# A convolution feeding two gated layers: the first two tiles convolved in PSUM with paired tails, and weight blocks split where they are first needed

## What is computed

```python
x_pad = np.concatenate([np.zeros((B, pad, D)), x], axis=1)
out = np.einsum('hk,bskhg->bshg', softmax(weight), x_unf)   # 7 taps
h = x @ w_in;  g = h * np.cos(h);                          x = g @ w_out   # layer 1
h = x @ w_in2; g = h * np.clip(h + 3.0, 0.0, 6.0) / 6.0;   out = g @ w_out2 # layer 2
```

## Time and profile before

| | us |
|---|---|
| median of 3 runs (2280.49 to 2280.93) | 2280.5 |
| the profiled execution | 2280.99 |
| its span, first to last instruction | 2279.3 |
| TensorE busy | 2245.0 (98%) |
| VectorE busy | 1811.7 (79%) |
| ScalarE busy | 1722.4 (76%) |
| GpSimd busy | 1509.4 (66%) |

### The profile page before, as it was taken

One profiled execution on the slowest core, in us unless ns is written; L12 is line 12 of the kernel. 1 busy time (PEld: TensorE's weight loads), 2 busy tenths in 40 slices (PEclk: granted clock), 3 DMA queues, 4 the chain that ended last, 5 costly groups with the idle time before them and its releaser, 6 DMA issues.

```text
span 2279.3 us, 56966 instructions
## 1 busy us (share of the span) xinstructions
PE 2245.0 (98%) x19560; PEld 1842.9 (81%) x19560; DVE 1811.7 (79%) x2509; ACT 1722.4 (76%) x2836; POOL 1509.4 (66%) x1059
## 2 busy tenths in 40 slices
PE   7899999999999999999999999999999999999998
PEld 5688888888888888888888888888888888888886
DVE  8778877888877887878888778888778878788753
ACT  5867777777777777777777777777777777777774
POOL 6766666667666667666666666676666676666664
PEclk9999999999999999999999999999999999999999
...
DMA packets 208245, 33.04 MB, mean 14 GB/s; under 512 B 203088, under 2 KB 207184, under 8 KB 208208
## 3 DMA queue, kind: packets, MB, share of 16 engines
...
## 4 chain that ended last, share of the span: by engine, by line
PE 94%; DVE 3%; ACT 2%; issue 0%; SPq 0%; DMA 0%; DVEq 0%; ACTq 0%
PE h_ps L390 45%; PE acc L397 30%; PE acc_tail L404 20%; ACT pre L562 1%; DVE gate L669 1%; DVE pre L658 1%; ACT g_hi L569 1%; DVE in_ftail L717 1%; DVE in_f L717 1%; ACT pre L552 0%; DVE in_tail L730 0%; DMA blk_tail<-in_x 0%; SPq L333 0%; ACT wout L598 0%; ACT in_hi L581 0%
## 5 line engine op out<-in xcount | busy, mean ns | idle before, releaser
L824 POOL TENSOR_TENSOR g_lo<-gate,g_hi 128x512 fp32r<-128x512 f32 x1024 | 1469.0, 1456 | 722.2 <-ACT g_hi L569 721.8
L397 PE MATMUL acc<-g_hi,wout 64*128 64x512 f32 x4096 | 1421.9, 387 | 1.7 <-POOL g_lo L824 1.7
L397 PEld LDWEIGHTS acc<-g_hi,wout 64*128 64x128 f32 x4096 | 755.0, 184 | 84.8 <-issue 3.4
L390 PE MATMUL h_ps<-in_hi,win_hi 64*128 64x512 f32 x2048 | 798.7, 391 | 11.8 <-DVE in_tail L730 10.7
L404 PE MATMUL acc_tail<-g_lo,wout 64*128 64x512 f32 x2048 | 797.6, 389 | 0.0
L390 PE MATMUL h_ps<-in_lo,win_hi 64*128 64x512 f32 x2048 | 792.9, 387 | 0.0
L390 PE MATMUL h_ps<-in_hi,win_lo 64*128 64x512 f32 x2048 | 792.9, 387 | 0.0
L390 PE MATMUL h_ps<-in_tail,wtail_hi 64*128 64x512 f32 x2048 | 792.7, 387 | 0.0
L404 PE MATMUL acc_tail<-g_hi,wout 64*128 64x512 f32 x2048 | 792.4, 387 | 0.0
L397 PE MATMUL acc<-g_lo,wout 64*128 64x512 f32 x2048 | 791.7, 387 | 0.0
L569 ACT ACTIVATE g_hi<-gate 128x512 fp32r<-128x512 f32 x1024 | 616.7, 631 | 116.0 <-DVE gate L672 56.8
...
## 6 DMA issues: line engine op xcount, KB each, us to landing
x_in<-in_x SPq DMA_DIRECT2D x128, 64.0 KB, 2.2
out_dram<-o_blk SPq DMA_DIRECT2D x128, 64.0 KB, 1.8
...
```

The costliest lines, as they stand in the source:

```text
L390: return pe.matmul(chunk_of(h_ps, q, half), w, x, start=start, stop=stop)
L397: return pe.matmul(acc[pair][:, :], wout[layer][rows, 2 * q + half, cols], g[rows, :], start=start, stop=stop)
L824: pool.tensor_tensor(chunk_of(g_lo, q, half), chunk_of(gate, q, half), chunk_of(g_hi, q, half).bitcast(F32), ALU.subtract).then_inc(glo_re ...
```

## The change

**Tiles 0 and 1.** `conv_first` puts the taps of tiles 0 and 1 into PSUM: main parts into acc[0] and acc[1], which are not in use yet, and the two tails, 64 rows each, together into acc_tail[1] with one instruction of 128 rows. Tile 1's tail is loaded early by ScalarE's queue into the lower half of blk_tail, and `turn_two_tails` transposes both. Tile 0's and the tails' taps come ahead of phase 0; tile 1's main taps (STEPS_1) lie in its slots 0 to 3. xT's leading halo is zeroed by a memset, and `keep_halo` copies only what later tiles need. x's main and tail have semaphores of their own. taps and head_of are widened so that the tail's tap values stand on 128 rows.

**Weights.** ORDER loads and splits the blocks as 0, 1, 4, 2, 3, 5, 6, ... Ahead of phase 0 ScalarE makes five high, and GpSimd four low. HIGH_IN and LOW_IN give the slot of each other block on each engine, through phases 0, 1 and 2, with GpSimd a slot behind or more. TensorE waits for the place of just the block that it needs.

**Hand-over.** SPLIT_EARLY, SPLIT_AFTER_DRAIN, CONV and the order of tail and twin in `split_high` change; of these SPLIT_EARLY and CONV[0] act in every turn.

**Warm-up.** 21 pairs, three after each convolution step from the seventh on, once block 0 is high.

```diff
-        stage_bufs = [stage[:, 0, :], stage[:, 1, :], pre[:, 0, :], pre[:, 1, :], gate[:, 0, :], gate[:, 1, :]]
+        ORDER = [0, 1, 4, 2, 3, 5] + list(range(6, 2 * BLOCKS))
+        stage_bufs = [pre[:, 0, :], gate[:, 0, :], pre[:, 1, :], gate[:, 1, :], stage[:, 0, :], stage[:, 1, :]]
...
-        STEPS = [(t, part) for t in range(TAPS) for part in (0, 1)]
+        HIGH_FIRST = ORDER[0:4]
+        HIGH_IN = {0: {0: 5, 2: 6, 4: 7, 6: 8}, 1: {0: 9, 2: 10, 5: 11}, 2: {0: 12, 2: 13, 4: 14, 6: 15}}
+        LOW_IN = {1: 3, 2: 5, 4: 6, 6: 7, 8: 8, 10: 9, 12: 10, 14: 11, 17: 12, 19: 13, 21: 14, 23: 15}
+
+        MAIN, TAIL = 0, 1
+        STEPS = [(t, part) for t in range(TAPS) for part in (MAIN, TAIL)]
+        STEPS_0 = [(0, MAIN), (1, MAIN)] + [s for t in range(TAPS - 2) for s in ((t, TAIL), (t + 2, MAIN))]
+        STEPS_0 += [(TAPS - 2, TAIL), (TAPS - 1, TAIL)]
+        STEPS_1 = [(t, MAIN) for t in range(TAPS)]
         DRAIN_SLOT = LAG
         SPLIT_SLOT = SLOTS - 3
         TURN_SLOT = SLOTS - 1
-        CONV_FIRST = [4, 4, 6, 8, 10, 12, 14, 14, 14]
-        CONV = {0: [0, 0, 1, 1, 1, 2, 2, 3, 4], 1: [4, 6, 8, 10, 11, 14, 14, 14, 14]}
+        CONV_FIRST = [0, 1, 3, 5, 7, 7, 7, 7, 7]
+        CONV_SECOND = [0, 0, 1, 2, 2, 2, 2, 3, 4]
+        CONV = {0: [0, 0, 0, 1, 1, 1, 2, 3, 4], 1: [4, 6, 8, 10, 11, 14, 14, 14, 14]}
+        TWIN_1, TAIL_1, LOW_TAIL_1, HIGH_1, LOW_1 = 1, 3, 4, 5, 5
         TURNS = 19
         L1, L2 = 0, 1
-        SPLIT_EARLY = {"hi": 1, "twin": 2, "tail": 4, "low_main": 2, "low_tail": 5}
-        SPLIT_AFTER_DRAIN = {"hi": 4, "twin": 4, "tail": 5, "low_main": 5, "low_tail": 6}
+        SPLIT_EARLY = {"hi": 0, "twin": 1, "tail": 2, "low_main": 1, "low_tail": 4}
+        SPLIT_AFTER_DRAIN = {"hi": 4, "twin": 4, "tail": 4, "low_main": 5, "low_tail": 5}
...
-
             def warm_up():
 
-                pe.wait_ge(whi_done, 2)
-                pe.wait_ge(conv_step, WARM_STEP)
-                for _ in range(2 * WARM_SERIES):
-                    warm_units(0, HALF_FF - 2 * P)
-                for _ in range(WARM_SERIES):
-                    warm_units(16, HALF_FF - 2 * P)
-                for _ in range(WARM_SERIES):
-                    warm_units(0, HALF_FF - 2 * P + 16)
-                for _ in range(WARM_SERIES):
-                    warm_units(16, HALF_FF - 2 * P + 16)
+                pe.wait_ge(whi_done, 1)
+                for n in range(WARM_STEP, len(STEPS_0)):
+                    pe.wait_ge(conv_step, n)
+                    for _ in range(WARM_PAIRS):
+                        for rows, half in ((LOW, 0), (UP, 1)):
+                            pe.matmul(chunk_of(h_ps, 1, half), win_hi[L1][rows, 0:P], win_hi[L1][rows, 0:TOK],
+                                      start=True, stop=True)
 
...
+                        weight_high(HIGH_IN[ph.setup][q])
+
+            for b in range(P // BLK, BLOCKS_D):
+                act.dma_start(chip_block(x_in, x_in_tail, b), dram_block(x_blocks, 0, b)).then_inc(x_tail_loaded, 16)
             act.wait_ge(w_step, 2)
             act.activation(w_soft[:, :], w_soft[:, :], ACT.Exp).then_inc(w_exp, 1)
 
+            for b in range(P // BLK, BLOCKS_D):
+                act.dma_start(chip_block(x_in, o_blk_tail, b),
+                              dram_block(x_blocks, 1, b)).then_inc(x_tail_loaded, 16)
             act.wait_ge(const_ready, CONSTS)
             act.activation(unused[:, :], half_pi[:, :], ACT.Sin)
-            for b in range(BLOCKS - 2):
+            for b in HIGH_FIRST:
                 weight_high(b)
-            act.wait_ge(conv_step, len(STEPS))
-            split_high(L1, L2)
-            for b in range(BLOCKS - 2, BLOCKS):
-                weight_high(b)
+            act.wait_ge(conv_step, STEPS_0.index((TAPS - 1, MAIN)) + 1)
+            split_hi(acc[0][:, :], L2)
+            act.wait_ge(conv_step, len(STEPS_0))
+            split_tail(acc_tail[1][0:DT, :], L2)
+            act.wait_ge(hi_ready[L2], 2)
+            split_twin(in_tail[L2][0:DT, :].bitcast(F32), L2)
+            weight_high(ORDER[4])
             phase(first_phase())
...
+            def turn_two_tails():
+
+                dve.wait_ge(x_tail_loaded, 16 * (BLOCKS_D - P // BLK) * 2)
+                dve.transpose(xT_tail[:, HALO:], blk_tail[:, :]).then_inc(x_tail_turned, 2)
 
             def turn_result(i, drained):
 
@@ -697,38 +736,73 @@
             def put_halo(i):
 
 
-                dve.wait_ge(x_turned, 2 * (i + 1))
-                for buf, kept in ((xT, halo), (xT_tail, halo_tail)):
+                dve.wait_ge(x_turned, i + 1)
+                dve.wait_ge(x_tail_turned, i + 1)
+                for buf, kept in ((xT, halo), (xT_tail[0:DT, :], halo_tail)):
                     dve.tensor_copy(buf[:, 0:HALO], halo_at(kept, i)).then_inc(halo_ready, 1)
                     dve.tensor_copy(halo_at(kept, i + B), buf[:, TOK:]).then_inc(halo_ready, 1)
 
+            def keep_halo(i):
+
+                dve.wait_ge(x_turned, i + 1)
+                rows = slice(i * DT, (i + 1) * DT)
+                dve.tensor_copy(halo_at(halo, i + B), xT[:, TOK:]).then_inc(halo_ready, 1)
+                dve.tensor_copy(halo_at(halo_tail, i + B), xT_tail[rows, TOK:]).then_inc(halo_ready, 1)
+
+            def tap(dst, src, scalar, t):
+
+                if t == 0:
+                    return dve.tensor_scalar(dst, src[:, t:t + TOK], scalar, None, ALU.mult)
+                return dve.scalar_tensor_tensor(out=dst, in0=src[:, t:t + TOK], scalar=scalar, in1=dst,
+                                                op0=ALU.mult, op1=ALU.add)
+
+            def conv_first(i, n):
+
+                steps = (STEPS_0, STEPS_1)[i]
+                t, part = steps[n]
+                if t > 0:
+                    dve.wait_ge(conv_step, steps_before(i) + steps.index((t - 1, part)) + 1)
+                elif part == TAIL:
+                    dve.wait_ge(x_tail_turned, 2)
+                else:
+                    dve.wait_ge(x_turned, i + 1)
...
                                   in_tail[to][0:DT, :].bitcast(F32), ALU.subtract).then_inc(lo_ready[to], 1)
+
+            def split_low_1(q):
+
+                if q == LOW_TAIL_1:
+                    dve.wait_ge(twin_ready[L1], 1)
+                    dve.tensor_tensor(in_tail[L1][DT:P, :], acc_tail[1][DT:P, :],
+                                      in_twin[L1][DT:P, :].bitcast(F32), ALU.subtract).then_inc(lo_ready[L1], 1)
+                    keep_halo(1)
+                if q == LOW_1:
+                    dve.wait_ge(hi_ready[L1], 2)
+                    dve.tensor_tensor(in_lo[L1][:, :], acc[1][:, :], in_hi[L1][:, :].bitcast(F32),
+                                      ALU.subtract).then_inc(lo_ready[L1], 1)
 
...
-            put_halo(1)
-            for n in range(CONV_FIRST[0]):
-                conv_taps(1, n)
+            for n in range(len(STEPS_0)):
+                if n == STEPS_0.index((0, TAIL)):
+                    turn_two_tails()
+                conv_first(0, n)
+            split_low_main(acc[0][:, :], L2, 0)
+            split_low_tail(acc_tail[1][0:DT, :], L2, 0)
+            keep_halo(0)
+            dve.wait_ge(halo_ready, 4)
+            turn_main(1)
             phase(first_phase())
-            for ph in turn_phases(1):
-                phase(ph)
-            with dve.Fori(2, TILES - 2) as k:
```

More of the change, by code:

```diff
@@ L18 @@
 WARM_STEP = 7
-WARM_SERIES = 10
+WARM_PAIRS = 3
 G_BUFS = 4
@@ L218, in staged_by @@
         def staged_by(b):
-            return 16 * sum(len(loads_of(a)) for a in range(b + 1) if buffer_of(a) == buffer_of(b))
+            return 16 * sum(len(loads_of(a)) for a in ORDER[:place(b) + 1] if buffer_of(a) == buffer_of(b))
         def every_other(a, rows, odd):
@@ L309, in turn_phases @@
             first = isinstance(k, int) and k == 1
+            second = isinstance(k, int) and k == 2
             last = isinstance(k, int) and k == TILES - 1
@@ L312, in turn_phases @@
             late = isinstance(k, int) and k + 2 >= TILES
-            return [Phase(L1, k, base, L1 if first else L2, 2 * k - 1, None, None, more, 1 if first else None, L1),
+            return [Phase(L1, k, base, L1 if first else L2, 2 * k - 1, None, None, more, 1 if first else 3 if second else None, L1),
                     Phase(L2, k - 1, base + SLOTS, L1, 2 * k, None if first else k - 2, None if late else k + 2,
@@ L532, in _ @@
             phase(first_phase())
-            for ph in turn_phases(1):
-                phase(ph)
-            with pe.Fori(2, TILES - 2) as k:
+            for k in (1, 2):
+                for ph in turn_phases(k):
+                    phase(ph)
+            with pe.Fori(3, TILES - 2) as k:
                 for ph in turn_phases(k):
@@ L639, in _ @@
+            act.wait_ge(hi_ready[L2], 2)
+            split_twin(in_tail[L2][0:DT, :].bitcast(F32), L2)
+            weight_high(ORDER[4])
             phase(first_phase())
-            for ph in turn_phases(1):
-                phase(ph)
```

(19 more changed lines are left out.)

208 lines of the change are left out of this document (107 added, 101 removed).

## The result

The changed kernel takes 2258.22 us (median, 2257.65 to 2259.22) against 2280.49 beside it: a ratio of 0.9903, 95% interval 0.9886 to 0.992. A later comparison gave 2257.71 and 0.9899 (0.9884 to 0.9914). The forecast was 2252 in a range of 2243 to 2264: the sign and the parts were right, and 6 of the 28 us expected did not come. The profiled execution took 2258.0 us, 23.0 less than that of before.

A forecast was written before the change was run, and what follows sets the result against it. It took a start-up in which TensorE waits and a loop that keeps it nearly always at work; 23.9 us won by phase 2's start and 4.9 in the loop made 2281.0 into 2252.2, range 2243 to 2264.

The forecast's parts named there:

- A: Start of phase 0: at 19.0 us instead of 29.76, 10.8 us gained, with bounds of 17.5 and 22.
- rival 2: Start-up dearer: tails land near 10 us, or TensorE idles before slot 3 and its clock falls; 2256 to 2261, chance 0.17.
- PSUM against SBUF: Ahead of phase 0: the two opening taps into PSUM run at single rate and cost 0.4 us more than in SBUF.
- B: Slot 0, from phase 0's start to slot 1's fraction: 8.3 us instead of 10.12, 1.8 us gained.
- C: Slots 1 to 14 of phases 0 and 1: 62.9 us instead of 67.56, 4.7 us gained.
- D: Hand-over to phase 2: it starts 2.3 us after slot 14's fraction instead of 9.0, 6.7 us gained.
- E: The loop: about 0.17 us of waiting per turn goes; over 29 turns 4.9 us, between 0 and 7.3.

The follow-up runs named there:

- run 3: The changed kernel with the first two tiles' taps written to SBUF instead of PSUM, same order and pairing of tails: 2267.33 us.
- run 4: The changed kernel with all eight blocks of layer 1 split ahead of phase 0 instead of slot by slot: 2260.96 us.
- run 1: The changed kernel with the old hand-over tables (SPLIT_EARLY and CONV[0]) put back: 2263.28 us.
- run 2: The kernel before the change with only the new SPLIT_EARLY and CONV[0]: 2275.97 us.
- run 9: The changed kernel itself, timed once more: 2257.71 us.
- run 6: The changed kernel with tile 1's two tail loads issued by SyncE between x's main part and the first weight block: 2254.81 us.
- run 10: The changed kernel with tile 1's tails issued by SyncE behind x's main part, tile 2's x loaded ahead of block 8, two warm-up pairs per step: 2254.1 us.
- run 5: The changed kernel with tile 1's two tail loads issued by ScalarE ahead of Exp: 2255.37 us.
- run 12: The changed kernel without any warm-up (WARM_PAIRS = 0): 2259.5 us.
- run 11: The kernel of run 10 with block 12's high and low parts split a slot earlier: 2255.18 us.

## Why the prediction was right, and where 6 us went

The four parts of the mechanism came out: taps in PSUM free of GpSimd (run 3), blocks split in the slots (run 4), the shorter turn (runs 1 and 2), and the shorter hand-over to phase 2, which is read from the intervals alone. No run takes back the pairing of the tails or phase 1's new order by itself. In the profiled executions the forecast was 2252.2 and the time 2258.0. Part by part:

- **A, start of phase 0: 21.76 instead of 19.0, 2.8 us short.** The step that failed is the landing of tile 1's tails: 8.0 taken from bounds of 6.7 and 10, measured 10.8 (joint transpose at 10.86, and at 11.10 in run 9), beyond both bounds. Part of this is the draw of one execution: of the eight joint transposes listed under run 9, seven are later than 8.0 and one is earlier (7.69). I took the value nearest to 2.33 us from issue to landing, "because another engine issues them than the weights". The issuing engine did not help: ScalarE's loads landed after 7.64 us behind SyncE's, and SyncE's own, issued ahead of the weights, were in use at 7.35 (run 6) and 7.65 (run 10). What differs is what is on the DMA engines by then. The Trainium skill says so (DMA: Bandwidth & Descriptors, Issuing engines are not separate DMA queues: loads of all issuing engines run on the same 16 and interleave), and I had not weighed it. The trace agrees. The view of the DMA engines, 0 to 12 us, after:

```profile
DMA  0000004899979899876996798958599999999999
...
blk_tail<-in_x ACTq DMA_DIRECT2D x4, 64.0 KB, 2.7
```

  The window has 40 slices of 0.3 us: from the eighth (2.1 us) on the DMA engines are mostly eight tenths busy or more. Of the four tail loads (two of each tile) the median is 2.7 us, but the last took 7.64. Runs 5 and 6 put the same loads ahead of the weights, and phase 0 came to 19.6 and 19.1. The case was in rival 2 (tails near 10, 2256 to 2261, chance 0.17), which is what happened; its other half, a clock that falls before slot 3, happened too, and cost nothing instead of 2 to 4 us. The rest of A held: ten steps at 0.66 (0.62 forecast), block four at 16.03. The warm-up did end after the low part (21.94 against 21.08 for the tail's low part), which cost 0.65; the forecast had it end 1.0 us ahead of them, from steps that the tails' landing has since moved. The clock stayed up into phase 0, as forecast.
- **PSUM against SBUF.** By the rows, an opening tensor_scalar into PSUM takes 0.75 us; into SBUF it takes 0.49 (run 3's first tap, and 492 ns in the earlier trace rows). The Trainium skill's rule (VectorE: DVE Perf Modes, Why PSUM operands drop a tier), taken for the destination, agrees. The 0.5 us for the two opening taps (0.4 by the prediction's reading) are drowned by the 7.1 us that run 3 shows on the other side.
- **B, slot 0: 8.45 us (21.76 to 30.21), forecast 8.3.** Right, and run 12 shows that 2.6 of it hang on the clock.
- **C, slots 1 to 14: 64.9 us, forecast 62.9, 2.0 short.** Slot 7 took 5.58 instead of 4.1: x of tile 2 is issued behind block 9, whose buffer GpSimd must free, and it lands 1.5 us after VectorE wants it. I had priced the added turning at nothing without following its load through SyncE's queue. Slot 4 took 5.70 instead of 5.2, since both of its halo copies were held. The other eleven are within 0.3 us of the forecast.
- **D, hand-over to phase 2: 2.38 us (95.10 to 97.48), forecast 2.3.** Right.
- **Two stalls that I did not have.** Phase 2 is 0.7 us longer than its 34.5, most of it at block 12 (0.44 us of standing still, and 0.11 more until the matmuls start 0.23 apart again). I had counted GpSimd's work in phase 2 (33.2 of 34.5 us) and costed it at nothing; here a queue so full delivered late, and run 11 shows that the stall can't be shifted away by one slot. Phase 3 is 0.4 us longer than before: its first four slots take 18.9 us by the fractions (137.80 to 156.72) where the loop's take 18.6, and in the seventh no matmul follows the one at 158.51 until 159.00, for a gate. The cause stays open.
- **E, the loop: 0.18 us per turn, 5.1 from the end of phase 3 on, forecast 4.9.** Right, by runs 1 and 2.

Summed: 2.8 + 0.15 + 2.0 + 0.1 + 0.7 + 0.4 - 0.2 is 5.95, against the 5.8 us that did not come; the rest is rounding.

One reading of the rows was off, and nothing hung on it: phase 0 of the kernel before did not start at the low clock. The clock granted fell at 30.6, and its first three matmuls start 0.33 and 0.24 us apart.

The best version run is 6 or 10, at 2254.8 and 2254.1 us, 3 to 4 us below the change; between these two the measurement doesn't decide.
